# Attention units aligned with the fourteen-step groups of the up-projection, on one Trainium2 core

## The reference

```python
kv  = einsum('bhsd,bhse->bhde', k, v)          # 8 heads of 64
out = einsum('bhsd,bhde->bhse', q, kv)
x   = out / sqrt(mean(out*out, -1) + 1e-6) * g_norm      # -> (8, 576, 512)
u   = x + low_rank(x)                          # U, V of rank 32 along the sequence
y   = u + relu(u @ w_ch1) @ w_ch2              # 512 -> 2048 -> 512
```

## Time and profile before

| | |
|---|---|
| three runs | 1354.85 us median (1354.66 to 1355.14) |
| the profiled execution's own time | 1356.87 us |
| its span, first to last instruction | 1355.1 us |
| TensorE busy | 1291.8 us, 95% |
| VectorE busy | 915.2 us, 68% |
| ScalarE busy | 521.4 us, 38% |
| GpSimd busy | 97.3 us, 7% |
| mean granted TensorE clock | 0.993 |

### The profile page before, as it was taken

How to read it: one execution, slowest core, us unless ns; L and a number is a source line. 1 busy time by engine, 2 the same in 40 slices (tenths; PEclk the granted TensorE clock), 3 DMA queues, 4 the chain that set the end, 5 groups by cost and what they waited for, 6 DMA issues and landing times.

```text
span 1355.1 us, 22351 instructions
## 1 busy us (share of the span) xinstructions
PE 1291.8 (95%) x8446; PEld 1238.0 (91%) x8446; DVE 915.2 (68%) x1300; ACT 521.4 (38%) x856; POOL 97.3 (7%) x107
## 2 busy tenths in 40 slices
PE   5789999999999998989999999999999999999998
PEld 5788999999999997989999999998898998988987
DVE  4977575656565659788889888895646446447443
ACT  4654434444443432545444454554312222222121
POOL 6220000000000000000000000000210111102100
PEclk9899999999999999999999999999999999999999
DMA  9444445454545425738346183634241350340421
GB/s 232 131 141 132 149 132 156 134 158 143 157 147 159 133 104 194 256 116 277 129 150 215 64 272 108 220 94 156 32 117 36 78 116 24 88 110 22 97 55 39
DMA packets 253831, 178.66 MB, mean 132 GB/s; under 512 B 165920, under 2 KB 224304, under 8 KB 253760
## 3 DMA queue, kind: packets, MB, share of 16 engines
q1 hardware_dynamic: 250800, 172.81, 42.8%
q0 software_dynamic: 1600, 4.56, 1.2%
q10 hardware_dynamic: 1360, 0.30, 0.1%
HBM read 109.47 MB, written 66.06 MB: 130 GB/s over the span
## 4 chain that ended last, share of the span: by engine, by line
PE 61%; issue 23%; DVE 8%; POOL 3%; ACT 3%; DMA 1%; SPq 1%; POOLq 0%; DVEq 0%; ACTq 0%
PE ps L1413 17%; PE ps L1415 17%; PE ps L1414 17%; PE ps L1434 2%; PE ps L1418 2%; PE ps L1442 2%; POOL rs L667 1%; POOL x_lo L661 1%; PE ps L1450 1%; DVE w L1031 1%; DVE h_st L1082 1%; ACT w L738 1%; PE ps L1461 1%; DVE y L998 1%; ACT y_hl L721 1%
## 5 line engine op out<-in xcount | busy, mean ns | idle before, releaser
L1413 PE MATMUL ps<-x_hi,w 128*128 128x288 f32 x896 | 273.0, 305 | 25.7 <-DVE h_st L1082 7.9
L1414 PE MATMUL ps<-x_lo,w 128*128 128x288 f32 x896 | 265.5, 296 | 0.0
L1415 PE MATMUL ps<-x_hi,w 128*128 128x288 f32 x896 | 265.1, 296 | 0.0
L1413 PE MATMUL ps<-r_hi,w_hi 128*128 128x384 f32 x672 | 225.0, 335 | 3.7 <-DVE r_lo L1210 2.7
L1414 PE MATMUL ps<-r_lo,w_hi 128*128 128x384 f32 x672 | 224.5, 334 | 0.0
L1415 PE MATMUL ps<-r_hi,w_lo 128*128 128x384 f32 x672 | 224.5, 334 | 0.0
L863 ACT ACTIVATE r_hi<-hb 128x768 fp32r<-128x768 f32 x168 | 142.2, 848 | 169.3 <-PE ps L1415 164.4
L1413 PEld LDWEIGHTS ps<-x_hi,w 128*128 128x128 f32 x896 | 169.6, 189 | 31.7 <-DVE h_st L1084 7.9
L1414 PEld LDWEIGHTS ps<-x_lo,w 128*128 128x128 f32 x896 | 169.8, 190 | 0.0
L1415 PEld LDWEIGHTS ps<-x_hi,w 128*128 128x128 f32 x896 | 169.8, 189 | 0.0
L1210 DVE TENSOR_TENSOR r_lo<-hb,r_hi 128x768 fp32r<-128x768 f32 x120 | 114.4, 956 | 34.5 <-ACT r_hi L863 34.5
(11 more groups left out here) (163 smaller groups left out, 2517.1 us busy)
## 6 DMA issues: line engine op xcount, KB each, us to landing
hT_scratch<-h_st SPq DMA_DIRECT2D x64, 576.0 KB, 4.6
hb<-hT_scratch SPq DMA_DIRECT2D x24, 1536.0 KB, 7.3
uT_scratch<-x_raw SPq DMA_DIRECT2D x32, 288.0 KB, 2.3
x_st<-uT_scratch SPq DMA_DIRECT2D x24, 384.0 KB, 3.7
x2T_scratch<-x_st SPq DMA_DIRECT2D x24, 384.0 KB, 6.9
x_raw<-x2T_scratch SPq DMA_DIRECT2D x8, 1152.0 KB, 5.8
xt_in<-x2T_scratch SPq DMA_DIRECT2D x144, 64.0 KB, 2.6
k_raw<-in_k SPq DMA_DIRECT2D x64, 128.0 KB, 3.0
```

What stands on the lines that cost most here:

```text
L1413: mm(dst, ws[0], xs[0], start=first, stop=False)
L1414: mm(dst, ws[0], xs[1], start=False, stop=False)
L1415: return mm(dst, ws[1], xs[0], start=False, stop=last)
```

## The change

`PERIOD` becomes 14, so that each unit takes one group. Attention of the next unit now stands behind step 11 of the group, the transposes behind step 1, low rank behind 4, `u_transposed` behind 8. Only tile 0 has an attention of its own at step 0; tile 6 has one attention less. On ScalarE the copy of the transposed q's main part stays behind the square root, its tail and the copies of kv go behind `a_part`. The sums and splits of x for the next tile, of which most stood between step 47 and the end, are spread: two sums and two low parts before the border, two sums and five low parts behind it (`x_then`). The addition that fills `c22` moves from idx 4 to behind the first addition of idx 5, so that the product of the next group waits for five additions in place of six. Tile 7's `x_high` and `x_low` follow the same new places.

```diff
-PERIOD, QK, LOW, UT = 12, 2, 8, 11
+PERIOD, QK, LOW, UT, ATT = 2 * NI, 1, 4, 8, 11
@@ ScalarE, up_tile
-            X_HIGH_AT = (HALF_UT + 2, HALF_UT + 4, LAST_UT + 4, LAST_UT + 5, LAST_UT + 8)
+            X_HIGH_AT = (23, 33, 53, 54)
+            X_HIGH_THEN = (5, 6, 7)
...
-                    if at_ == 0:
+                    if first and k == 0:
                         attn_copy(m, BX, BY)
                         squares(m, sq)
-                    elif at_ == QK:
+                    if at_ == QK:
                         std(m)
                         if more:
                             q_copy(m + 1, BX)
                     elif at_ == QK + 1:
                         y_high(m)
-                    elif at_ == QK + 2 and more:
-                        act.wait_ge(s_kv, m + 2)
-                        q_copy_tail(m + 1, BY)
-                        kv_copy(m + 1, BY, P)
-                    elif at_ == LOW:
+                    elif at_ == LOW + 1:
                         a_part(m, BX)
+                        if more:
+                            act.wait_ge(s_kv, m + 2)
+                            q_copy_tail(m + 1, BY)
+                            kv_copy(m + 1, BY, P)
                     elif at_ == UT:
                         u_evacuated(m, r, BX, 1 - par, t)
+                    elif at_ == ATT and more:
+                        attn_copy(m + 1, BX, BY)
+                        squares(m + 1, sq)
+                    if k in X_HIGH_THEN and not first:
+                        x_high(t, par, 4 + X_HIGH_THEN.index(k))
@@ VectorE, added (idx 4, then idx 5)
-                    dve.wait_ge(s_ad, NADD * n + 3)
-                    nc.vector.tensor_tensor(c22, c21, c22, ALU.add).then_inc(s_ad, 1)
                 elif idx == 5:
                     dve.wait_ge(s_ad, NADD * n + 4)
                     nc.vector.tensor_tensor(c12, p, c12, ALU.add).then_inc(s_ad, 1)
+                    nc.vector.tensor_tensor(c22, c21, c22, ALU.add).then_inc(s_ad, 1)
@@ VectorE, up_tile
+            def x_then(t, par, k, first=False):
+
+                if k == 0 and not first:
+                    x_sum(t, par, 6)
+                elif k in (1, 3) and not first:
+                    x_low(t, par, 2 + k // 2)
+                elif k == 4 and not first:
+                    x_sum(t, par, 4)
+                elif k in (5, 7, 8):
+                    x_low(t, par, 4 + (5, 7, 8).index(k))
...
-                    if at_ == 2:
+                    if at_ == 0:
                         sums(m, sq)
-                    elif at_ == 3:
+                    elif at_ == 1:
                         normalise(m)
-                    elif at_ == 4:
+                    elif at_ == 3:
                         y_low(m)
-                    elif at_ == LOW:
+                    elif at_ == LOW + 2:
                         a_split(m, BX)
-                    if k == HALF_UT + 1:
+                    x_then(t, par, k, first)
+                    if k == 32:
                         x_sum(t + 1, 1 - par, 1)
-                    if k == HALF_UT + 9:
-                        x_low(t + 1, 1 - par, 0)
-                    if k == LAST_UT + 2:
+                    if k in (33, 54):
+                        x_low(t + 1, 1 - par, (33, 54).index(k))
+                    if k == 52:
                         x_sum(t + 1, 1 - par, 2)
...
@@ TensorE, attention_step and up_step
-                if at_ == 0:
+                if first and k == 0:
                     pe.wait_ge(s_uev, m)
                     attention(m, BX, BY)
...
+                elif at_ == ATT and more:
+                    pe.wait_ge(s_uev, m + 1)
+                    attention(m + 1, BX, BY)
...
-                        pe.wait_ge(s_ad, NADD * (n - 1) + (6, 7, 3)[idx])
+                        pe.wait_ge(s_ad, NADD * (n - 1) + (5, 7, 3)[idx])
```

More of the change, by code:

```diff
@@ L36 @@
 NX = NI + 2
-PERIOD, QK, LOW, UT = 12, 2, 8, 11
-LAST_UT = (HP - 1) * PERIOD + UT
-HALF_UT = PERIOD + UT
+PERIOD, QK, LOW, UT, ATT = 2 * NI, 1, 4, 8, 11
 TT = 768
@@ L72, in hook @@
 def hook(k):
-    r, at_ = divmod(k, PERIOD)
-    return (r, at_) if r < HP else (HP, -1)
+    return divmod(k, PERIOD)
 def x_slot(idx, par):
@@ L806, in up_tile @@
                         copied(t, k)
-                    if k < 2 and not first:
-                        x_high(t, par, 5 + k)
                     if first and g + 1 < NG and idx in (2, 5) and s_ == 1:
@@ L879, in last_up_tile @@
                         copied(t, k)
-                    if k < 2:
-                        x_high(t, 1, 5 + k)
+                    if k in X_HIGH_THEN:
+                        x_high(t, 1, 4 + X_HIGH_THEN.index(k))
                     if k == 16:
@@ L1114, in _ @@
             w1_sums(dve, nc.vector, 1)
-            X_LOW_AT = (0, 1, 4)
+            def x_then(t, par, k, first=False):
[7 more added lines that the diff above has]
+                    x_low(t, par, 4 + (5, 7, 8).index(k))
             def up_tile(t, par, first=False, end=False):
@@ L1122, in up_tile @@
                         added(t, k)
-                    if k in X_LOW_AT:
-                        x_low(t, par, 4 + X_LOW_AT.index(k))
                     if first and g + 1 < NG and idx in (3, 6) and s_ == 0:
@@ L1128, in up_tile @@
                     m = HP * (t + 1) + r
-                    if at_ == 2:
+                    if at_ == 0:
                         sums(m, sq)
+                    elif at_ == 1:
+                        normalise(m)
                     elif at_ == 3:
-                        normalise(m)
-                    elif at_ == 4:
                         y_low(m)
-                    elif at_ == LOW:
+                    elif at_ == LOW + 2:
                         a_split(m, BX)
-                    if k == HALF_UT + 1:
+                    x_then(t, par, k, first)
+                    if k == 32:
                         x_sum(t + 1, 1 - par, 1)
-                    if k == HALF_UT + 9:
-                        x_low(t + 1, 1 - par, 0)
-                    if k == LAST_UT + 2:
+                    if k in (33, 54):
+                        x_low(t + 1, 1 - par, (33, 54).index(k))
+                    if k == 52:
                         x_sum(t + 1, 1 - par, 2)
-                    if k == LAST_UT + 3:
-                        x_sum(t + 1, 1 - par, 6)
-                    if k == LAST_UT + 4:
-                        x_low(t + 1, 1 - par, 1)
-                    if k == LAST_UT + 6:
-                        x_sum(t + 1, 1 - par, 4)
-                        x_low(t + 1, 1 - par, 2)
-                x_low(t + 1, 1 - par, 3)
             up_tile(0, 0, first=True)
@@ L1217, in last_up_tile @@
                         added(t, k)
-                    if k in X_LOW_AT:
-                        x_low(t, 1, 4 + X_LOW_AT.index(k))
+                    x_then(t, 1, k)
                     if k in (14, 15, 16, 18):
@@ L1488, in _, with attention_step @@
             u_transposed(3, 4, y_first[0])
-            def attention_step(k, t, end):
+            def attention_step(k, t, first, end):
                 r, at_ = hook(k)
@@ L1495, in attention_step @@
                 more = r + 1 < HP or not end
-                if at_ == 0:
+                if first and k == 0:
                     pe.wait_ge(s_uev, m)
                     attention(m, BX, BY)
-                elif at_ == QK and more:
+                if at_ == QK and more:
                     pe.wait_ge(s_o, 2 * (m + 1))
@@ L1544, in up_tile @@
                     if not final:
-                        attention_step(k, t, end)
+                        attention_step(k, t, first, end)
             up_tile(0, 0, first=True)
```

## The result

The change takes 1347.58 us (median of four runs, 1345.65 to 1348.15); the kernel before, run beside it, 1354.99 (1354.66 to 1355.64, four runs). The ratio is 0.9942 with a 95% interval of 0.9925 to 0.9959: faster by 0.6%, 7.4 us, where 16 were forecast. The profiled execution has 1347.18 of its own and a span of 1345.4, 9.7 us less than the span before.

A forecast was written before the change was run, and what follows sets the result against it. TensorE was taken to bound the kernel, with its waits to be won. Tiles 1 to 6 at -20.0 us and tile 0 at +4.0 gave -16.0, from 1354.85 to 1339 us; range 1331 to 1349.

The forecast's parts named there:

- Attention: Tiles 1 to 6: an undrawn wait at three of a tile's four attentions, 0.87 us in all, goes.
- Additions: TensorE's waits for VectorE's additions of products 5 and 6, 1.29 and 1.11 us a tile, both go.
- The chain: From attention to low rank, with seven steps and the transposes between: slack 0.15 us, no stall, but thin.
- B: Chain from attention to low rank late by some tenths: 28 units lose 7 to 12.6 us, 1346 to 1352; chance 0.14.
- D: Slower: chain from attention to low rank late by over 0.47 us past the slack, 16 lost in all; chance 0.07.
- The tile of 61.9: Each of tiles 1 to 5 takes 61.9 us: 61.5 plus 0.4 for small waits.
- The two small waits: Product 4 in a tile's first group waits 0.12 + 0.10 us; `u_transposed` in the third, 0.11 + 0.10.
- rival C: Waits only move: work on x stalls each tile's first group by 2.4 us; about 1352 to 1354, chance 0.09.
- Drawn idle understates: Tiles 1 to 6 hold 12.7 us by drawn idle, 19.6 by start times; drawn idle would forecast near 1348.
- the term of +4.0: Tile 0 loses: attention +1.1, unit 0 +4.0, unit 2 +2.1, less 3.2, gives +4.0 us; bounds -2 and +8.
- Tile 6: Without the transposes (1.66 us) and the last attention (1.11), tile 6 takes 59.1 us.
- A tile without any of these is 61.5: A tile of 64.75 us less stalls of 1.29, 1.11 and 0.87 takes 61.5 us.

The follow-up runs named there:

- the three edits together: The changed kernel with tile 0's weight split in the gaps, the loop written out and tile 6's last low rank two steps later: 1332.46 us, ratio 0.9815.

## Why the prediction fell short

The direction held, and 1347.6 lies inside the range, but of the forecast 16 us 7.4 came. The spans miss it by 6.3 us (9.7 in place of 16.0); the rest, 2.3, is the step from the profiled execution to the median, below.

**What held.** *Attention*: the undrawn wait is gone: the step ahead of attention starts at 269.10 in tile 3, attention at 269.90, 0.80 behind it. *Additions*: with room for them no wait for L1082 or L1084 is left but the one with the wrong name; and the two experiments on parts show that neither the additions alone bring that, nor alignment and additions without the spread sums of x. *The chain*: in the same tile `y_low` starts at 277.15 and takes 0.82, so it ends 0.27 ahead of low rank at 278.24; less the 0.1 taken for the hand-over that is 0.17 of slack, forecast 0.15. Rivals B and D are out, and the run with the sums at the border shows what they would have cost. *The tile of 61.9*: tile 5 has 61.85, and all five have 61.86 without the loop. The two small waits that it holds are there, undrawn: in tile 3 of the version written out, by start times, the step ahead of product 4 and the one behind it take 0.25 more together than 0.80 each (forecast 0.22), and the one ahead of the third group's `u_transposed` 0.15 (forecast 0.21). That is far from the 2.4 us a tile of rival C. *Drawn idle understates*: in tiles 1 to 6 it was 13.4 us before, and with the three edits together, where none is left, the stretch is 20.3 shorter, of which the attention that left tile 6 is 1.1. The prediction gave "near 1348" by the drawn idle; its own two sums, 12.7 and 19.6, differ by 6.9, which gives 1346, and that the time came out at 1347.6 is luck.

**Tile 0, the term of +4.0, was mis-sized: it measured +8.2.** The waits it names are there: `a_split` behind the weight block in three units, 7.8 us in all. What was missing is what goes with them in the clock. The half-clock pieces in tile 0 last 17.9 us and cost 8.9 after the change, 8.2 and 4.1 before; that is +4.9, and without it the tile would be at +3.3. Of the 4.9, two more falls behind `u_transposed` than before are 3.4 and the piece at 53.02 is 1.7; the start gives 0.3 back. The step had the clock as a bound only ("+8 if the clock falls once more as often as it did here"), and the centre should have taken it: before the change already, the mean of 0.95 stood beside stalls, and the step added longer ones. Cutting GpSimd's sums or moving the blocks shortened the stalls, and with them two or all three of the falls behind `u_transposed` went.

That the clock answers to the stall is read from these coincidences; no run held the stalls and changed the clock. In the profiles a fall stands behind each of the three stalls of 1.92 to 3.00 us after the change; with the sums cut, those of 1.74 and 1.25 are followed by none, that of 1.92 by one. The length alone does not tell: before the change, of two stalls in tile 0 the shorter has a fall at its end, in the piece from 81.13, and the longer has none:

```profile
81.47 0.66 PE L1418 MATMUL ps<-identF,y 128*128 128x128 f32 x2 [2.24 <-DVE a_aug L1011]
...
109.37 0.40 PE L1413 MATMUL ps<-x_hi,w 128*128 128x288 f32 x1 [2.53 <-DVE w L1031]
```

Single profiles of tile 0 also differ with no edit in it: 83.79 in place of 85.61 in the change with its loop written out, 79.31 in place of 77.42 in the kernel before with its loop written out. Of the 4.2 us by which this term missed, about 2 are thus no more than the difference between two profiles of the same tile.

That the waits came near their forecast in sum is in part luck. Unit 0, forecast at 4.0 from the end of GpSimd's last sum, waited 2.83: the sums ended at 63.20, before `a_split` began, and what came late was the low part and the weight block that they had lengthened. Unit 1, whose wait was taken as unchanged, went from 2.24 to 3.00, and the largest wait stood there and not in unit 0.

**Tile 6 was mis-sized by 1.5 us.** The step took off the transposes of 1.66 us and the attention, but the chain's slack of 0.15 was worked out with those transposes between attention and low rank. Without them the last unit waits 1.66 - 0.15 = 1.5: its wait of 1.3 drawn, the one for `y_hl`. The run with low rank two steps later took it away.

**The loop was not in the sum.** "A tile without any of these is 61.5" counted every border alike. The jump back at the border of tiles 2 and 3 costs 1.8 us, and tiles 1, 3 and 4 are some 0.25 to 0.33 longer each: 2.65 against the version written out. In the kernel before only 0.57 of the jump showed, in tile 2's 65.33 against 64.75.

**The median.** The change was carried from a profiled execution 2.0 us above its median; that of after stands 0.4 below its own. The step assumed that the difference stays, and 2.4 us of the miss are in it. (As a gain it is 2.3, since the kernel before, run beside the change, stood 0.14 above the median that the forecast started from.) With more runs, beside the experiments, the kernel before lies at 1355.9 to 1356.8, nearer to its profiled execution than to the three runs. That three runs were too few is the likely reading; what sets an execution apart from the next stays open.

Tile 0 +4.2, tiles 1 to 6 +4.0, and -1.8 for tile 7, the rest and the start, which were forecast unchanged: +6.4, the spans' miss to 0.1. No run looks into the -1.8, which hid part of the miss.

## What to carry to other kernels

A stall that goes can uncover another at the same place, so ask of each what else arrives there just behind it: here a loop's jump, and a chain that only the transposes had covered. An operation moved off one wait can also lengthen another elsewhere, as the moved addition did at step 44. Where a term of the sum adds stalls of some us to the matrix engine in a stretch whose granted clock is already below 1.00, put the clock's loss into the centre, not only into the bounds. Parts that bring nothing to the time by themselves (the additions alone, or the alignment with the additions) can bring the gain once the last part is there, so undo parts one at a time from both ends.

## What the runs showed that was not expected

A loop of two turns (some 970 matmuls a turn on TensorE, some 130 operations on VectorE) costs TensorE 1.8 us at its one jump back, and 0.25 to 0.33 us in each of the other tiles inside, once nothing hides it; the trace puts the wait down to an addition that TensorE does not wait for. GpSimd loses by the contention as well: its fourth sum in unit 1 of tile 0 took 2.93 us where others of its size take 1.30, and before the change the third of unit 0 took 3.07, so both engines are slower while both work.
